# Bucketed attention with two MLPs: the clamp of the scores on VectorE becomes a row maximum, and ScalarE's exponential reads the scores from PSUM

## The chip, the cores and the metric

The kernel runs on one core of one Trainium2 chip. The metric is the device time of one execution in microseconds (us); the median of three runs stands for it. A core has TensorE (matrix products and transposes into PSUM, called PE), VectorE (DVE), ScalarE (ACT), GpSimd (POOL), and SyncE (SP), which here only starts DMA transfers. Each engine runs its own instructions in order, and the engines meet through semaphores.

## The reference, cut to what matters

```
mask   = q_bucket[:, :, :, None] == k_bucket[:, :, None, :]      # buckets: signs of 6 projections
scores = scale * q @ k.T ;  scores = where(mask, scores, -1e9)
scores = scores - max(scores, axis=-1) ;  attn = exp(scores) / (sum(exp(scores)) + 1e-9)
x = (attn @ v)  as (B*S, H*D)            # B 2, H 8, S 768, D 64
x = rational(x @ w_in0) @ w_out0         # 1536 x 512 -> 2048 -> 512, a cubic over a quadratic
x = (h * relu6(h + 3) / 6) @ w_out1      # h = x @ w_in1, the same sizes
```

A query whose bucket holds no key has -1e9 in its whole row, so its attention is uniform.

## The kernel before, in words

There are 16 heads, taken as 8 pairs, and each head has 6 tiles of 128 queries by 768 keys: 96 tiles, numbered n here, with j = 0 to 11 inside a pair and t = 0 to 5 inside a head. The 96 tiles are 96 steps, written out by hand in the same order on every engine. What one tile goes through is:

- **scores (L799 to L813)**: PE computes a tile of scores into one of two PSUM buffers (`s_ps`, by j % 2) with four products. Queries and keys are split in a high and a low part. The bits of the bucket stand as extra rows of `q_main` and `k_main`, so that a query and a key in different buckets get 2^33 per differing bit. All signs are turned: `q_main` and `q_cross` hold queries times -1/8 (`scale_col`), so the wanted maximum is a minimum.
- **clamp (L603)**: DVE reads the tile, takes the smaller of it and 1e9, writes it to `probs` in SBUF, and gets the row minimum (`least`) as accumulator output. `scores(n)` waits for `clamped` of tile n-2, since it writes the same buffer.
- **exponentials (L430)**: ACT computes exp(least - probs) in place in `probs`, with the row sum.
- **invert (L611)** on DVE, **normalise (L386)** on POOL: probs times 1 / row sum. `alone` is a wait followed by an increment of a semaphore that nobody reads.
- **turn_probs (L815)**: PE transposes tile n-3 in two halves of three 128 x 128 blocks; `take_turned` on ACT (first half) and on DVE (second half) copies them to SBUF.
- **weigh (L823)**: PE multiplies the transposed tiles of the pair before with v, spread over the steps: two k-blocks at t = 3, one at t = 1, 2, 4 and 5, none at t = 0. The first pair has no weigh at all. `upper_x` (ACT) and `lower_x` (DVE) split the result into `x_hi` and `x_lo`, which frees the bank for the next group.

A step on PE is: scores(n), a part of weigh, at j = 0 the projections of the next pair (`project`), then turn_probs(n-3). A step on DVE is: clamp(n), invert(n-1), at t = 0 lower_x, take_turned(n-3), at j = 1 `threshold` (the bits of the next pair), at t = 3 `split_lo` (the low parts of head h+2). A step on ACT is: at t = 0 upper_x, exponentials(n-1), take_turned(n-3), at t = 2 `split_hi` of head h+2, and in pairs 3 to 6 at j = 7 and j = 10 the high part of a weight (`split_weights`). A step on POOL is: normalise(n-1), and in pairs 3 to 6 at j = 8 and j = 11 the low part of a weight. In the last pair weigh is placed by `LAST_WEIGH` (L50): none at j = 0, 5, 10 and 11.

After the 96 steps the two MLPs follow in three chunks of 512 tokens each, with PE products back to back (L842 to L911). The diff does not touch them. Their first hidden products wait for the last exponentials and share PSUM banks with the scores.

Of the kernel before, what the change touches and what calls it, by code (L numbers as in the profile page):

```python
# [23 lines left out]
ALU = mybir.AluOpType  # L24
# [5 lines left out]
PENALTY = 2.0 ** 33  # L30
MASKED = 1e9


def bucket_attention_and_two_mlps(nc, q, k, v, proj, w_in0, w_out0, poly_a, poly_b, w_in1, w_out1, out):
# [57 lines left out]
    with ctx:  # L92
# [19 lines left out]
        three_col = sb("three_col", [P, 1])  # L112
        least = sb("least", [P, 4])
        scale_col = sb("scale_col", [P, 1])
        row_sum = sb("row_sum", [P, 4])
# [50 lines left out]
        sel_made = sem("sel_made")  # L166
        scale_made = sem("scale_made")
        proj_made = sem("proj_made")
# [13 lines left out]
        scored = sem("scored")  # L182
        clamped = sem("clamped")
        exped = sem("exped")
# [172 lines left out]
        def _(pool):  # L357
# [7 lines left out]
            def below(c, limit, fill):  # L365
# [5 lines left out]
            nc.gpsimd.memset(bit_sel[:, 0, :], TINY).then_inc(sel_made, 1)  # L371
            nc.gpsimd.memset(bit_sel[:, 1, :], -1.0).then_inc(sel_made, 1)
            pool.wait_ge(sel_made, 2)
# [3 lines left out]
            below(0, 3 * BITS, TINY)  # L377
            below(1, QUAD, -1.0)
            nc.gpsimd.memset(ident[:, :], 0.0).then_inc(sel_made, 1)
# [3 lines left out]
            nc.gpsimd.affine_select(out=ident[:, :], in_=ident[:, :], compare_op=ALU.not_equal, fill=1.0,  # L383
                                    base=0, pattern=[[-1, P]], channel_multiplier=1).then_inc(sel_made, 1)

            def normalise(n, j):  # L386
# [12 lines left out]
            for i in range(PAIRS):  # L399
                for j in range(2 * TILES):  # L400
                    n = 2 * TILES * i + j
                    if n >= 1:
                        normalise(n - 1, j - 1)
                    if early_half(i, j - 1):
                        f, half = early_half(i, j - 1)
                        split_weights(0, f, (half,))
# [8 lines left out]
        def _(act):  # L415
# [6 lines left out]
            def split_hi(h):  # L422

                i, u = divmod(h, 2)
                act.wait_ge(raw_in[i % 2][u], 32 * (i // 2 + 1))
                after(act, scored, TILES * (h - SETS + 1))
                nc.scalar.activation(q_main[h % SETS][:, :], raw[i % 2][u][:, :], ACT.Identity,
                                     scale=scale_col[:, 0:1]).then_inc(hi_made, 1)

            def exponentials(n, j):  # L430
                r = j % 4
                act.wait_ge(clamped, n + 1)
                nc.scalar.activation(probs[r][:, :], probs[r][:, :], ACT.Exp, scale=-1.0, bias=least[:, r:r + 1],  # L433
                                     accum_out=row_sum[:, r:r + 1]).then_inc(exped, 1)
# [141 lines left out]
        def _(dve):  # L576
            nc.vector.memset(proj_pair[:, :], 0.0).then_inc(proj_made, 1)
            nc.vector.memset(scale_col[0:D, :], -SCALE).then_inc(scale_made, 1)
            nc.vector.memset(scale_col[D:P, :], 1.0).then_inc(scale_made, 1)
            dve.wait_ge(proj_in, 32)  # L580
# [14 lines left out]
            def split_lo(h):  # L595

                c = h % SETS
                dve.wait_ge(hi_made, h + 1)
                nc.vector.scalar_tensor_tensor(q_cross[c][:, :], raw[h // 2 % 2][h % 2][:, :], scale_col[:, 0:1],
                                               q_main[c][:, :].bitcast(F32), ALU.mult, ALU.subtract)\  # L600
                    .then_inc(lo_made, 1)

            def clamp(n, j):  # L603

                r = j % 4
                dve.wait_ge(scored, n + 1)
                after(dve, turned, 2 * (n - 3))
                nc.vector.tensor_scalar(probs[r][:, :], s_ps[j % 2][:, 0:SEQ], MASKED, None, ALU.min, ALU.min,  # L608
                                        accum_out=least[:, r:r + 1]).then_inc(clamped, 1)

# [21 lines left out]
            def step(i, j):  # L632
                h, n = 2 * i + j // TILES, 2 * TILES * i + j
                t = j % TILES
                clamp(n, j)
                if n >= 1:
# [9 lines left out]
                if t == 3 and h + 2 < NHEAD:  # L646
# [3 lines left out]
            nc.vector.tensor_reduce(bit_col[:, :], bit_sel[:, :, :], AX.X, ALU.min).then_inc(bit_col_made, 1)  # L650
            dve.wait_ge(scale_made, 2)
            dve.wait_ge(raw_in[0][0], 32)
            nc.vector.tensor_scalar(q_main[0][:, :], raw[0][0][:, :], scale_col[:, 0:1], None, ALU.mult)\
                .then_inc(first_q, 1)
            dve.wait_ge(first_q, 1)
# [4 lines left out]
            dve.wait_ge(swapped_in, 32)  # L660
            nc.vector.tensor_scalar(q_cross[0][D:P, :], swapped[D:P, :], -SCALE, None, ALU.mult).then_inc(first_q, 1)
            nc.vector.scalar_tensor_tensor(q_cross[0][0:D, :], raw[0][0][0:D, :], -SCALE,
                                           q_main[0][0:D, :].bitcast(F32), ALU.mult, ALU.subtract).then_inc(first_q, 1)
            dve.wait_ge(first_q, 4)
# [117 lines left out]
        def _(pe):  # L782
# [16 lines left out]
            def scores(h, i, u, n, j, t):  # L799
# [5 lines left out]
                if n == 0:  # L805
                    pe.wait_ge(first_k, 2)
                after(pe, clamped, n - 1)
                rows = slice(P * t, P * (t + 1))
# [157 lines left out]
```

## Time and profile before

| | us |
|---|---|
| median of 3 runs | 774.07 (773.98 to 776.07) |
| the profiled execution, its own time | 773.98 |
| its span | 772.2 |
| PE busy | 751.7 (97%) |
| DVE busy | 484.8 (63%) |
| ACT busy | 431.7 (56%) |
| POOL busy | 170.0 (22%) |

The profile was taken from one execution. Its span leaves 1.8 us of that execution's time outside. A busy share is an average over stages: attention takes the first 240 us, the first MLP the stretch to about 510 us, the second one the rest. In the chain of work that ended last PE has 93% of the span.

### The profile page before, as it was taken

What the parts mean: (1) busy time and instruction counts of PE and PEld (TensorE: products, weight loads), DVE (VectorE), ACT (ScalarE), POOL (GpSimd) and SP (SyncE); (2) the same over time, 40 slices, a digit from 0 to 9 for tenths busy, and PEclk for the clock granted to TensorE, in tenths of its full rate; (3) what the DMA queues carried; (4) which work ended last, traced back from release to release, by engine and by line L of the source; (5) the groups of instructions that cost most, each with busy time, mean ns of one, the idle gap of its engine ahead of it and who ended that gap; (6) DMA issues with size and microseconds to landing.
All of it is one profiled execution on the core that took longest, in us unless ns stands there. A gap on an engine that the chain in (4) does not pass through costs nothing.

```text
span 772.2 us, 10988 instructions
## 1 busy us (share of the span) xinstructions
PE 751.7 (97%) x3712; PEld 580.0 (75%) x3712; DVE 484.8 (63%) x892; ACT 431.7 (56%) x783; POOL 170.0 (22%) x174
## 2 busy tenths in 40 slices
PE   4799999999999999999999999999999999999998
PEld 2666666666666888888888888888888888888886
DVE  4977777777766788899888998852222322232223
ACT  2866676776756888777676889852222221212121
POOL 0433344544531354200000244530000000000000
PEclk9999999999999999999999999999999999999999
DMA  6644355445300333100000133320000100010001
GB/s 149 161 119 108 89 135 136 94 108 126 80 27 1 83 86 105 56 0 0 0 0 0 42 96 109 89 76 0 1 1 0 54 0 0 0 55 0 1 1 55
DMA packets 35082, 43.29 MB, mean 56 GB/s; under 512 B 4192, under 2 KB 23392, under 8 KB 35040
## 3 DMA queue, kind: packets, MB, share of 16 engines
q1 hardware_dynamic: 34752, 42.32, 20.5%
q10 hardware_dynamic: 288, 0.43, 0.2%
q8 instruction: 24, 0.39, 0.2%
q14 instruction: 18, 0.15, 0.1%
HBM read 26.61 MB, written 3.15 MB: 39 GB/s over the span
## 4 chain that ended last, share of the span: by engine, by line
PE 93%; DVE 3%; DMA 1%; ACT 1%; issue 1%; SPq 1%; ACTq 0%; DVEq 0%
PE y_ps L911 34%; PE h_ps L857 11%; PE h_ps L858 11%; PE h_ps L859 11%; PE o_ps L837 9%; PE t_ps L820 8%; PE s_ps L810 3%; PE s_ps L811 3%; DVE probs L608 2%; DMA probs<-in_k 1%; DVE x_lo L629 1%; PE p_ps L794 1%; PE p_ps L837 1%; ACT probs L433 1%; DMA k_cross<-q_cross 0%
## 5 line engine op out<-in xcount | busy, mean ns | idle before, releaser
L703 DVE SCALAR_TENSOR_TENSOR t_abs<-t_abs,h_ps 128x512 f32<-128x512 f32 x48 | 33.0, 688 | 187.2 <-ACT t_abs L504 187.2
L857 PE MATMUL h_ps<-x_hi,slot 128*128 (+1 forms) x384 | 149.7, 390 | 0.0
L858 PE MATMUL h_ps<-x_lo,slot 128*128 (+1 forms) x384 | 149.4, 389 | 0.0
L859 PE MATMUL h_ps<-x_hi,slot 128*128 (+1 forms) x384 | 149.4, 389 | 0.0
L504 ACT ACTIVATE t_abs<-h_ps,three_col 128x512 f32<-128x512 f32 x48 | 33.1, 690 | 191.8 <-PE h_ps L859 191.8
L396 POOL TENSOR_TENSOR slot<-w_raw,slot 128x512 fp32r<-128x512 f32 x64 | 81.6, 1295 | 207.7 <-ACT slot L459 207.7
L911 PE MATMUL y_ps<-g_hi,slot 128*128 128x512 f32 x384 | 126.1, 389 | 0.0
L911 PE MATMUL y_ps<-slot,g_hi 128*128 128x512 f32 x384 | 118.3, 389 | 0.0
L389 POOL TENSOR_SCALAR probs<-probs,row_inv 128x768 f32<-128x768 f32 x96 | 87.2, 908 | 138.4 <-DVE row_inv L613 138.0
L820 PEld LDWEIGHTS t_ps<-ident,probs 128*128 128x128 f32 x576 | 61.9, 141 | 51.6 <-issue 34.3
L608 DVE TENSOR_SCALAR_CACHE_REDUCE probs<-s_ps 128x768 f32<-128x768 f32 x96 | 91.6, 954 | 12.6 <-PE s_ps L811 6.2
L433 ACT ACTIVATE probs<-probs,least 128x768 f32<-128x768 f32 x96 | 89.4, 931 | 10.8 <-DVE probs L608 10.7
L820 PE MATMUL t_ps<-ident,probs 128*128 128x128 f32 x576 | 84.1, 281 | 4.4 <-DVE pt_second L623 2.0
L857 PEld LDWEIGHTS h_ps<-x_hi,slot 128*128 128x128 f32 x384 | 72.1, 188 | 15.6 <-issue 0.6
L911 PEld LDWEIGHTS y_ps<-g_hi,slot 128*128 128x128 f32 x384 | 72.1, 188 | 15.3 <-DVE g_lo L709 0.2
L911 PEld LDWEIGHTS y_ps<-slot,g_hi 128*128 128x128 f32 x384 | 72.1, 188 | 14.9
L859 PEld LDWEIGHTS h_ps<-x_hi,slot 128*128 128x128 f32 x384 | 72.1, 188 | 14.9
L858 PEld LDWEIGHTS h_ps<-x_lo,slot 128*128 128x128 f32 x384 | 72.1, 188 | 14.8
L810 PE MATMUL s_ps<-k_cross,q_cross 128*128 128x512 f32 x192 | 74.3, 387 | 3.7 <-DMA k_main<-bits 2.9
L911 PE MATMUL y_ps<-g_lo,slot 128*128 128x512 f32 x192 | 74.7, 389 | 0.0
L911 PE MATMUL y_ps<-slot,g_lo 128*128 128x512 f32 x192 | 74.7, 389 | 0.0
L837 PE MATMUL o_ps<-pt_first,v_nat 128*64 128x384 f32 x180 | 72.8, 506 | 1.8 <-DVE x_lo L629 1.8
(72 smaller groups left out, 1097.9 us busy)
## 6 DMA issues: line engine op xcount, KB each, us to landing
w_raw<-in_moe_w_in SPq DMA_DIRECT2D x32, 256.0 KB, 2.7
w_raw<-in_moe_w_out SPq DMA_DIRECT2D x32, 256.0 KB, 2.7
raw<-in_q SPq DMA_DIRECT2D x16, 192.0 KB, 3.2
v_nat<-in_v SPq DMA_DIRECT2D x16, 192.0 KB, 3.1
raw<-in_k SPq DMA_DIRECT2D x15, 192.0 KB, 3.5
k_main<-q_main SPq DMA_DIRECT2D x15, 192.0 KB, 2.6
k_cross<-q_main SPq DMA_DIRECT2D x15, 192.0 KB, 3.1
k_cross<-q_cross SPq DMA_DIRECT2D x15, 192.0 KB, 2.6
```

Source lines behind the costliest of these rows:

```text
L389: nc.gpsimd.tensor_scalar(probs[j % 4][:, :], probs[j % 4][:, :], row_inv[:, r:r + 1], 1.0, ALU.mult, ALU.mult).then_inc(normed, 1)
L396: nc.gpsimd.tensor_tensor(slots[f][:, j, 1, :], w_raw[j][:, :], slots[f][:, j, 0, :].bitcast(F32), ALU.subtract).then_inc(w_lo_made, 1)
L433: nc.scalar.activation(probs[r][:, :], probs[r][:, :], ACT.Exp, scale=-1.0, bias=least[:, r:r + 1], accum_out=row_sum[:, r:r + 1]).then_in ...
L504: nc.scalar.activation(t_abs[b][:, :], h_ps[b][:, :], ACT.Relu, bias=three_col[:, :])\
L608: nc.vector.tensor_scalar(probs[r][:, :], s_ps[j % 2][:, 0:SEQ], MASKED, None, ALU.min, ALU.min, accum_out=least[:, r:r + 1]).then_inc(cla ...
L810: mm(s_ps[j % 2][:, c0:c1], q_cross[c][:, rows], k_cross[c][:, c0:c1], start=True, stop=False)
L820: last = nc.tensor.transpose(t_ps[half][:, P * s:P * (s + 1)], probs[n % 4][:, c:c + P], ident[:, :])
L837: last = mm(weigh_bank(e)[D * u:D * (u + 1), 0:HALF], v_nat[i % 2][u][:, kt, :], pt(i, u, g)[:, kt, :], start=(kt == 0), stop=(kt == TILES ...
L857: mm(h_ps[b][:, :], w_hi, x_hi[:, kt, cols], start=(kt == 0), stop=False)
L858: mm(h_ps[b][:, :], w_hi, x_lo[:, kt, cols], start=False, stop=False)
L859: last = mm(h_ps[b][:, :], w_lo, x_hi[:, kt, cols], start=False, stop=(kt == KT - 1))
L911: last = mm(y_ps[d][:, :], still, moving, start=(f == 0 and a == 0), stop=(f == FT - 1 and a == 2))
```

## The change: what it does

The signs are turned back: queries are copied unscaled, the bits of the query side are 1 instead of -1, and the score is large and negative outside the bucket. DVE no longer rewrites the tile: `maximum(n)` reads the PSUM buffer and writes one number per row, minus the row maximum (`neg_max`). Two new POOL instructions of one column, `bias(n)`, stand ahead of normalise(n-1) in POOL's order: the first makes `exp_scale` = 1/8 where the row has a key in its bucket (`neg_max` under 2^32) and 0 where not, the second makes `exp_bias` = `neg_max` times `exp_scale`. ACT's exponential now reads the scores in PSUM, with both as operands of one number per row, and writes `probs`. It takes over the wait for a free `probs` buffer (tile n-4 transposed). `scores(n)` waits for `exped` of tile n-2 instead of `clamped`. `split_hi` becomes a copy without a scale, `split_lo` a subtraction without one; two memsets of `scale_col` go. MATCHED is 2^32.

```diff
-MASKED = 1e9
+MATCHED = PENALTY / 2
@@ POOL
-            nc.gpsimd.memset(bit_sel[:, 1, :], -1.0).then_inc(sel_made, 1)
+            nc.gpsimd.memset(bit_sel[:, 1, :], 1.0).then_inc(sel_made, 1)
-            below(1, QUAD, -1.0)
+            below(1, QUAD, 1.0)
+            def bias(n, j):
+                r = j % 4
+                neg = neg_max[:, r:r + 1]
+                alone(maxed, n + 1)
+                nc.gpsimd.tensor_scalar(exp_scale[:, r:r + 1], neg, MATCHED, SCALE, ALU.is_lt, ALU.mult)\
+                    .then_inc(matched, 1)
+                alone(matched, n + 1)
+                nc.gpsimd.tensor_scalar(exp_bias[:, r:r + 1], neg, exp_scale[:, r:r + 1], 1.0, ALU.mult, ALU.mult)\
+                    .then_inc(biased, 1)
...
+                    bias(n, j)
                     if n >= 1:
                         normalise(n - 1, j - 1)
@@ ACT
-                nc.scalar.activation(q_main[h % SETS][:, :], raw[i % 2][u][:, :], ACT.Identity,
-                                     scale=scale_col[:, 0:1]).then_inc(hi_made, 1)
+                nc.scalar.activation(q_main[h % SETS][:, :], raw[i % 2][u][:, :], ACT.Copy).then_inc(hi_made, 1)
...
-                act.wait_ge(clamped, n + 1)
-                nc.scalar.activation(probs[r][:, :], probs[r][:, :], ACT.Exp, scale=-1.0, bias=least[:, r:r + 1],
+                act.wait_ge(biased, n + 1)
+                after(act, turned, 2 * (n - 3))
+                nc.scalar.activation(probs[j % 4][:, :], s_ps[j % 2][:, 0:SEQ], ACT.Exp,
+                                     scale=exp_scale[:, r:r + 1], bias=exp_bias[:, r:r + 1],
                                      accum_out=row_sum[:, r:r + 1]).then_inc(exped, 1)
@@ DVE
-                nc.vector.scalar_tensor_tensor(q_cross[c][:, :], raw[h // 2 % 2][h % 2][:, :], scale_col[:, 0:1],
-                                               q_main[c][:, :].bitcast(F32), ALU.mult, ALU.subtract)\
-                    .then_inc(lo_made, 1)
+                nc.vector.tensor_tensor(q_cross[c][:, :], raw[h // 2 % 2][h % 2][:, :], q_main[c][:, :].bitcast(F32),
+                                        ALU.subtract).then_inc(lo_made, 1)
...
-            def clamp(n, j):
-                r = j % 4
-                dve.wait_ge(scored, n + 1)
-                after(dve, turned, 2 * (n - 3))
-                nc.vector.tensor_scalar(probs[r][:, :], s_ps[j % 2][:, 0:SEQ], MASKED, None, ALU.min, ALU.min,
-                                        accum_out=least[:, r:r + 1]).then_inc(clamped, 1)
+            def maximum(n, j):
+                dve.wait_ge(scored, n + 1)
+                nc.vector.tensor_reduce(neg_max[:, j % 4:j % 4 + 1], s_ps[j % 2][:, 0:SEQ], AX.X, ALU.max,
+                                        negate=True)\
+                    .then_inc(maxed, 1)
@@ PE
-                after(pe, clamped, n - 1)
+                after(pe, exped, n - 1)
```

The four instructions with which DVE makes the first head's operands lose their scale in the same way (a copy or a plain subtraction in place of each).

## Rows read from the trace of the kernel before

**Rows 1.** Busy time by stretch: busy us of each engine, clock, DMA share, GB/s.
```profile
20.00:30.00 10.00, 7.18 (x47) 6.00 (x48) 9.56 (x22) 7.50 (x16) 4.67 (x6) 1.00 0.67 181
70.00:100.00 30.00, 29.77 (x189) 19.28 (x187) 23.18 (x56) 20.64 (x43) 11.81 (x13) 1.00 0.45 112
```
**Rows 2.** Timeline of PE, first pair: start, us, then the instruction.
```profile
21.88 0.50 PE L810 MATMUL s_ps<-k_cross,q_cross 128*128 128x512 f32 x1 [0.83 <-DVE probs L608]
...
28.23 0.48 PE L810 MATMUL s_ps<-k_cross,q_cross 128*128 128x512 f32 x1
...
29.74 0.48 PE L810 MATMUL s_ps<-k_cross,q_cross 128*128 128x512 f32 x1
...
37.32 0.48 PE L810 MATMUL s_ps<-k_cross,q_cross 128*128 128x512 f32 x1
```
**Rows 3.** Timeline of DVE, first pair.
```profile
20.87 0.95 DVE L608 TENSOR_SCALAR_CACHE_REDUCE probs<-s_ps 128x768 f32<-128x768 f32 x1
...
22.92 0.16 DVE L613 RECIPROCAL row_inv<-row_sum 128x1 f32<-128x1 f32 x1 [0.16 <-ACT probs L433]
...
23.45 1.55 DVE L599 SCALAR_TENSOR_TENSOR q_cross<-raw,scale_col,q_main 128x768 fp32r<-128x768 f32 x1
24.93 0.94 DVE L608 TENSOR_SCALAR_CACHE_REDUCE probs<-s_ps 128x768 f32<-128x768 f32 x1
...
30.73 0.96 DVE L608 TENSOR_SCALAR_CACHE_REDUCE probs<-s_ps 128x768 f32<-128x768 f32 x1
```
**Rows 4.** Timeline of ACT, DVE and POOL around one exponential.
```profile
45.40 0.92 ACT L433 ACTIVATE probs<-probs,least 128x768 f32<-128x768 f32 x1
46.45 0.17 DVE L613 RECIPROCAL row_inv<-row_sum 128x1 f32<-128x1 f32 x1 [0.27 <-ACT probs L433]
46.81 0.91 POOL L389 TENSOR_SCALAR probs<-probs,row_inv 128x768 f32<-128x768 f32 x1 [1.40 <-DVE row_inv L613]
```
**Rows 5.** Timeline of POOL at the start: small instructions.
```profile
0.82 0.10 POOL L372 MEMSET bit_sel<- 128x4 f32 x1
0.99 0.19 POOL L367 TENSOR_SCALAR_AFFINE_SELECT bit_sel<-bit_sel 128x4 f32<-128x4 f32 x1
...
2.15 0.29 POOL L383 TENSOR_SCALAR_AFFINE_SELECT ident<-ident 128x128 f32<-128x128 f32 x1
```
**Rows 6.** Groups by line and shape, 36 to 268 us: count, busy us, mean ns.
```profile
L389 POOL TENSOR_SCALAR probs<-probs,row_inv 128x768 f32<-128x768 f32 x87 | 79.0, 908 | 114.4 <-DVE row_inv L613 113.9
...
L501 ACT ACTIVATE t_num<-h_ps,a_col 128x512 f32<-128x512 f32 x5 | 3.8, 765 | 0.0
...
L500 ACT ACTIVATE r_ps<-h_ps 128x512 f32<-128x512 f32 x5 | 3.0, 591 | 0.0
```
**Rows 7.** Timeline of DVE at the start: a single-source operation on 768 columns.
```profile
5.63 0.62 DVE L653 TENSOR_SCALAR q_main<-raw,scale_col 128x768 fp32r<-128x768 f32 x1 [1.75 <-DMA raw<-in_k]
```
**Rows 8.** Timeline of DVE, PE and ACT, second head of pair 1.
```profile
48.86 0.95 DVE L608 TENSOR_SCALAR_CACHE_REDUCE probs<-s_ps 128x768 f32<-128x768 f32 x1
...
51.78 0.48 PE L810 MATMUL s_ps<-k_cross,q_cross 128*128 128x512 f32 x1
...
52.49 0.94 ACT L433 ACTIVATE probs<-probs,least 128x768 f32<-128x768 f32 x1
...
53.16 0.47 PE L810 MATMUL s_ps<-k_cross,q_cross 128*128 128x512 f32 x1
...
54.34 0.54 PE L837 MATMUL o_ps<-pt_first,v_nat 128*64 128x384 f32 x1 [0.23 <-DVE x_lo L629]
55.77 0.48 PE L810 MATMUL s_ps<-k_cross,q_cross 128*128 128x512 f32 x1
56.66 0.54 PE L837 MATMUL o_ps<-pt_first,v_nat 128*64 128x384 f32 x1
```
**Rows 9.** Waits of PE in all: us in total, times, longest.
```profile
PE o_ps L837 <- DVE x_lo L629: 1.8, 8, 0.2
```
**Rows 10.** Timeline of PE at the end of attention.
```profile
233.11 0.47 PE L810 MATMUL s_ps<-k_cross,q_cross 128*128 128x512 f32 x1
```

More of the change, by code:

```diff
@@ L112, in bucket_attention_and_two_mlps @@
         three_col = sb("three_col", [P, 1])
-        least = sb("least", [P, 4])
-        scale_col = sb("scale_col", [P, 1])
+        neg_max = sb("neg_max", [P, 4])
+        exp_scale = sb("exp_scale", [P, 4])
+        exp_bias = sb("exp_bias", [P, 4])
         row_sum = sb("row_sum", [P, 4])
@@ L166, in bucket_attention_and_two_mlps @@
         sel_made = sem("sel_made")
-        scale_made = sem("scale_made")
         proj_made = sem("proj_made")
@@ L182, in bucket_attention_and_two_mlps @@
         scored = sem("scored")
-        clamped = sem("clamped")
+        maxed = sem("maxed")
+        matched = sem("matched")
+        biased = sem("biased")
         exped = sem("exped")
@@ L577, in _ @@
             nc.vector.memset(proj_pair[:, :], 0.0).then_inc(proj_made, 1)
-            nc.vector.memset(scale_col[0:D, :], -SCALE).then_inc(scale_made, 1)
-            nc.vector.memset(scale_col[D:P, :], 1.0).then_inc(scale_made, 1)
             dve.wait_ge(proj_in, 32)
@@ L634, in step @@
                 t = j % TILES
-                clamp(n, j)
+                maximum(n, j)
                 if n >= 1:
@@ L650, in _ @@
             nc.vector.tensor_reduce(bit_col[:, :], bit_sel[:, :, :], AX.X, ALU.min).then_inc(bit_col_made, 1)
-            dve.wait_ge(scale_made, 2)
             dve.wait_ge(raw_in[0][0], 32)
-            nc.vector.tensor_scalar(q_main[0][:, :], raw[0][0][:, :], scale_col[:, 0:1], None, ALU.mult)\
-                .then_inc(first_q, 1)
+            nc.vector.tensor_copy(q_main[0][:, :], raw[0][0][:, :]).then_inc(first_q, 1)
             dve.wait_ge(first_q, 1)
@@ L660, in _ @@
             dve.wait_ge(swapped_in, 32)
-            nc.vector.tensor_scalar(q_cross[0][D:P, :], swapped[D:P, :], -SCALE, None, ALU.mult).then_inc(first_q, 1)
-            nc.vector.scalar_tensor_tensor(q_cross[0][0:D, :], raw[0][0][0:D, :], -SCALE,
-                                           q_main[0][0:D, :].bitcast(F32), ALU.mult, ALU.subtract).then_inc(first_q, 1)
+            nc.vector.tensor_copy(q_cross[0][D:P, :], swapped[D:P, :]).then_inc(first_q, 1)
+            nc.vector.tensor_tensor(q_cross[0][0:D, :], raw[0][0][0:D, :], q_main[0][0:D, :].bitcast(F32),
+                                    ALU.subtract).then_inc(first_q, 1)
             dve.wait_ge(first_q, 4)
```

## The prediction

> **What bounds the kernel now.** I read the busy shares by stretch first. From 70 to 100 us, which stands for pairs 1 to 7, PE is busy 29.77 us of 30; in the first pair, 20 to 30 us, it is 7.18 of 10 while DVE has 9.56 [rows 1]. So attention has two regimes: a first pair without weigh, bound by DVE and by the passing of tiles between engines, and seven pairs bound by PE. Behind attention PE runs without gaps, with products the diff doesn't touch; what attention loses is not made up there. Then I read timelines, to see what each tile waits for. Scores of one tile start at 28.23 us and of the next at 29.74: 1.5 us a step where nothing special intervenes [rows 2]. In the steady part a usual step is 2.3 us long, but the second head's first tile, at 51.78, has no weigh and is followed by the next at 53.16, after 1.38 us [rows 8].
>
> **The new loop.** A PSUM buffer used to be free when DVE had clamped it. Now scores(n+2) waits for scores(n), row maximum, two POOL instructions and exponential in series. Its terms:
>
> - Start of scores to start of DVE's pass: 29.74 to 30.73, 0.99 us [rows 2, 3].
> - The pass: the clamp takes 0.95 [rows 3]. No reduction of that size from PSUM is in the trace. It reads the same 768 columns, so I take 0.95 again; the lower bound is the 0.62 of a single-source pass over 768 columns in SBUF [rows 7], the upper about 1.0.
> - POOL, from the end of the pass to the start of the exponential, called E. DVE to POOL through `alone`: the reciprocal ends at 46.62, normalise starts at 46.81, 0.19 [rows 4]. POOL has no one-column tensor_scalar to read. Below it stands a memset of 0.10; a select of 4 columns takes 0.19 and one of 128 columns 0.29 [rows 5]. That slope, 0.10 over 124 columns, makes 0.62 over 768, so of the 0.908 of normalise [rows 6] at most 0.29 is fixed cost. I take 0.22 an instruction, near the 4-column select. Between the two, POOL waits for itself: 0.07 from the memset's end at 0.92 to the select at 0.99 [rows 5] at least, 0.19 at most; I take 0.12. To ACT 0.05. Sum: 0.19 + 0.22 + 0.12 + 0.22 + 0.05 = 0.80. The ends are 0.19 + 0.10 + 0.07 + 0.10 + 0.05 = 0.51 and 0.19 + 0.29 + 0.19 + 0.29 + 0.08 = 1.04.
> - The exponential until PE may start: 45.40 to 46.45 when the reciprocal starts behind it, 1.05 [rows 4]. The second one-number-per-row operand adds: a pass over 512 columns takes 0.591 without any and 0.765 with two [rows 6], 0.087 each. So 1.05 + 0.08 = 1.13.
>
> Loop: 0.99 + 0.95 + 0.80 + 1.13 = 3.87 us for two steps, 1.93 from the end of the maximum. Where two steps on PE take less, PE waits.
>
> The Trainium skill, GPSIMD Engine Reference, section 3.1 on cycle accounting, has one- and two-operation bodies at 1.03 cycles per element at 1.2 GHz. By that, 768 columns are 0.66 us of the 0.908 and 0.25 is fixed, an estimate from that page; E would be 0.86 and the loop 3.93. No run here shows which of the two splits holds.
>
> **First pair.** Before, tile 2's clamp starts at 20.87, held up by the threshold that waits for a DMA, and scores of tile 4 start at 21.88 [rows 2, 3]. Nothing before that moves the 20.87. After: 20.87 + 0.95 = 21.82, plus 1.93 gives 23.75, 1.9 us late. Next, DVE's split_lo at t = 3 stands behind invert(2), which needs exponential 2: 21.82 + 0.80 + 1.05 = 23.67, where it was 22.92. From that reciprocal to the next clamp are 2.01 us (22.92 to 24.93), in which split_lo takes 1.55 [rows 3]. So maximum 4 starts at 25.68, ends at 26.63, and tile 6 starts at 28.56. Two loops later tile 10 starts at 28.56 + 7.74 = 36.30. For tile 12: tile 8 starts at 32.43, its exponential at 32.43 + 0.99 + 0.95 + 0.80 = 35.17, the reciprocal at 36.22, maximum 10 at 38.23 (split_lo again), its end 39.18, and tile 12 at 41.11. It was 37.32 [rows 2]: **+3.8 us**. E enters five times: the low end gives 2.3, the high end 5.0. The odd tiles stand between: their bias is queued behind a normalise of 0.91 on POOL, which delays it past the even tile's, but a loop of theirs is as long, so they follow at the same period. Up to 1.0 goes off if split_lo doesn't meet POOL's normalise as it seems to now (twice some 0.5).
>
> **Pairs 1 to 7.** A usual pair of steps on PE is 4.6 us, over the 3.87: no wait. Two places are tight. First, the short step: the exponential at 52.49 is held by ACT's own queue (copy, upper_x), not by E (tile j = 5's maximum would be ready at 51.41 + 0.80). Scores at 53.16 must now wait for it: 52.49 + 1.13 = 53.62, 0.46 late. The weigh behind starts 0.89 after its scores (55.77 to 56.66), so at 54.51; it stood at 54.34 because it waited 0.23 for x_lo [rows 8]. That leaves 0.17. PE has 8 such waits [rows 9], one a pair and a second in the last: 8 x 0.17 = **+1.4**. The ninth short step ends at 233.11 [rows 10] with no weigh behind it: its 0.46 falls partly into waits for DVE's copies at the end; I take **+0.2**. Second, the tile after split_lo: its maximum starts at 48.86 and ends at 49.81; + 1.93 is 51.74, and its PE step starts at 51.78 [rows 8]. That costs nothing, with 0.04 of room, twice in each pair. With E at 1.04 it costs 0.2 each of 14 times, 2.8.
>
> **The rest.** normalise(n-1) stands behind bias(n), but its reciprocal stood behind clamp(n) on DVE anyway; it comes 0.6 us later and is wanted two steps later, over 3 us in the short case: nothing. The POOL weight splits in pairs 3 to 6 delay the next bias by some 0.5, in steps with 0.7 of room: nothing. ACT's split_hi loses an operand (0.087) and DVE's split_lo too; they are off the path except once ahead of the first scores: -0.1. DVE loses the write of probs, which nobody waits for. SP's queue keeps its order; its key and bit transfers start up to 2 us later in the first pair, with several in hand. The last exponential is 0.9 later, and the last transposes stand behind 3 us of hidden products and a whole weigh. DVE's four first-head instructions: 0 within 0.1.
>
> Sum: 3.8 + 1.4 + 0.2 - 0.1 = +5.3 us on an execution of 773.98 (the median is 774.07, the same within 0.1): **779.3 us**. Own range, by E, the pass and the split_lo meeting: 776.6 to 783.
>
> **Rivals.**
>
> *POOL's small instructions are dearer, E about 1.04.* First pair +5.0, the tight places after split_lo +2.8, short steps as before 1.5: 783.3. For: normalise allows 0.29 fixed. Against: the 4-column select at 0.19. It decides above E = 0.84. Chance 0.17.
>
> *Not slower: the chain shrinks under DVE's own pace.* If the reduction, which writes no tile, runs like the 0.62 row less its fixed part, say 0.55, with E at 0.51 and the exponential at 1.05 (its PSUM source paying for the operand), the loop is 0.99 + 0.55 + 0.51 + 1.05 = 3.10, 1.55 a step against 1.5. invert(2) is then at 22.90, no later than now, tile 12 about 0.2 late; the short steps give 8 x 0.08 = 0.6. Place: the maximum and POOL; point: a loop under some 3.2 us. Time 774.7. Against: 0.95 for the clamp of the same tile. Chance 0.10. The Trainium skill, VectorE: DVE Perf Modes, the perf-mode tier table, gives tensor_reduce only the single rate, SBUF or PSUM; by it the pass stays at 0.95 and this case loses its main term. No row here shows a long reduction.
>
> *PE slows in the thinner first pair.* The granted clock reads 1.00 there [rows 1], but PE would be busy some 6 of 10 us. If products fall to half speed, scores take 0.65 more in each of five loops: +3.3, 782.6. Against: at 7.18 of 10 they stay at 0.48. Chance 0.06.
>
> **How the numbers follow.** Forecast 0.64, the three rivals 0.17, 0.10 and 0.06, unnamed gains 0.03. A measurement of this kernel tells about 0.3%, 2.3 us, from no change. Slower by more: forecast 0.62, rivals 0.23, so 0.85. Within: 0.02 of the forecast's low end and the not-slower rival, 0.12. Faster 0.03. Range 776.3 to 783.6.
>
> **What would show it.** Right: PE waiting for ACT at the scores of the first pair; two even tiles 3.9 us apart there; tile 12 at about 41 us; PE waiting for ACT 0.46 once a pair, at the second head's second tile, and a weigh behind it without a wait for DVE; POOL's two instructions near 0.2 each and 0.8 from L608's successor to the exponential; the MLPs' length unchanged. Wrong: waits of PE in usual steps or after split_lo (E too low), a reduction far from 0.95, or a first pair that ends before 39 us. The forecast falls if the first pair's period stays near 1.5.

## The result, and the profile after

The changed kernel takes **782.49 us** (782.09 to 783.22 over four runs), the kernel before 774.05 beside it (773.98 to 776.07). The ratio is 1.0103, 95% interval 1.009 to 1.0115: slower by 8.4 us. The prediction was 779.3, range 776.3 to 783.6. The sign and most of the places were right, and the size was too small by 3.2 us. The profiled execution spans 780.8 us, 8.6 more than that of before.

The table follows one thing through attention: by how much scores of a tile start later than in the kernel before. Each entry is the difference of two start times in the two timelines of PE. "Key split" is short for `split_lo`, the DVE instruction `q_cross<-raw,q_main`, which makes the low parts of a later head; it stands twice in each pair, in the last pair not at all. A "short step" is a step of PE without a weigh: one in each of pairs 1 to 6, at the pair's middle, and two in the last pair before its end.

| Where | later by, us | forecast |
|---|---|---|
| tile 12 (end of the first pair) | 4.40 | 3.8 |
| six short steps, pairs 1 to 6, after the weigh: 0.20 to 0.23 each | +1.36 | 6 x 0.17 = 1.0 |
| tile behind the second key split of a pair, pairs 1 and 2: 0.10 each | +0.20 | 0 |
| the same place, pairs 3 to 6: 0.44, 0.40, 0.43, 0.45 | +1.73 | 0 |
| last pair, its two short steps | +0.6 | 0.3 |
| end of attention | +0.4 | 0.2 |

The entries add up to 8.7 and the span grew by 8.6: between these places single tiles drift back by some hundredths. The tile behind the first key split of each pair is 0.10 late as well, but the short step comes right behind it and swallows that: its exponential is held by ACT's own queue, so the step costs 0.20 to 0.23 with that delay (here) and without it (experiment 1). Everything after attention has the length it had, 535.8 us from the first hidden product to the end against 535.7.

The two stretches of the busy table, to be held against [rows 1]; the columns are window, length, busy us of PE, PEld, DVE, ACT and POOL, granted clock, DMA share, GB/s:

```profile
20.00:30.00 10.00, 8.48 (x38) 7.33 (x39) 7.40 (x14) 6.54 (x13) 6.47 (x13) 1.00 0.66 181
70.00:100.00 30.00, 29.87 (x190) 19.32 (x191) 22.87 (x43) 21.66 (x45) 17.44 (x40) 1.00 0.41 98
```

DVE, which was 9.56 busy of the first ten, is now 7.40 busy. The first pair is no longer bound by one engine but by the series of PE, DVE, POOL and ACT that each buffer passes through. PE does fewer instructions in the same ten microseconds (38 against 47) and is busier: some of them ran at half rate, on which more below.

The loop of the first pair, in the timelines of POOL and ACT, and PE's answer to it [rows 2]:

```profile
26.85 0.23 POOL L394 TENSOR_SCALAR exp_scale<-neg_max 128x1 f32<-128x1 f32 x1 [0.68 <-DVE neg_max L618]
27.28 0.27 POOL L397 TENSOR_SCALAR exp_bias<-neg_max,exp_scale 128x1 f32<-128x1 f32 x1 [0.20 <-POOL exp_scale L394]
...
27.58 0.99 ACT L448 ACTIVATE probs<-s_ps,exp_bias,exp_scale 128x768 f32<-128x768 f32 x1 [0.75 <-POOL exp_bias L397]
...
28.81 0.47 PE L819 MATMUL s_ps<-k_cross,q_cross 128*128 128x512 f32 x1 [0.43 <-ACT probs L448]
```

From the exponential's start to PE's is 28.81 - 27.58 = 1.23 here; in most tiles of the first pair it is 1.13. The reduction before it starts at 25.70 and ends at 26.65, so E, from the end of the maximum to the exponential, is 27.58 - 26.65 = 0.93. It reads 0.92 to 0.93 wherever nothing else holds the exponential. The groups by shape give the parts:

```profile
L448 ACT ACTIVATE probs<-s_ps,exp_bias,exp_scale 128x768 f32<-128x768 f32 x96 | 95.0, 990 | 32.9 <-POOL exp_bias L397 31.5
L618 DVE TENSOR_REDUCE neg_max<-s_ps 128x1 f32<-128x768 f32 x96 | 91.6, 954 | 18.1 <-PE s_ps L820 15.0
...
L397 POOL TENSOR_SCALAR exp_bias<-neg_max,exp_scale 128x1 f32<-128x1 f32 x96 | 26.2, 273 | 19.9 <-POOL exp_scale L394 17.1 <-DVE row_inv L624 2.8
L394 POOL TENSOR_SCALAR exp_scale<-neg_max 128x1 f32<-128x1 f32 x96 | 21.6, 225 | 81.2 <-DVE neg_max L618 79.9
```

The short step, beside [rows 8]: scores at 56.34 and then 58.09, where 51.78 and 53.16 stood, and a weigh with no bracket behind it, so nothing to wait for.

```profile
56.34 0.47 PE L819 MATMUL s_ps<-k_cross,q_cross 128*128 128x512 f32 x1
...
56.95 1.00 ACT L448 ACTIVATE probs<-s_ps,exp_bias,exp_scale 128x768 f32<-128x768 f32 x1
...
58.09 0.51 PE L819 MATMUL s_ps<-k_cross,q_cross 128*128 128x512 f32 x1
...
59.01 0.54 PE L846 MATMUL o_ps<-pt_first,v_nat 128*64 128x384 f32 x1
```

PE's waits in all: the row of [rows 9], for x_lo, is gone, and this one has come.

```profile
PE s_ps L819 <- ACT probs L448: 6.1, 13, 1.3
```

**What the prediction called nothing.** Beside the ninth tile of a pair POOL splits a half of the next weights (L410), in pairs 3 to 6 only. POOL first, then DVE:

```profile
121.43 1.27 POOL L410 TENSOR_TENSOR slot<-w_raw,slot 128x512 fp32r<-128x512 f32 x1
122.67 0.23 POOL L394 TENSOR_SCALAR exp_scale<-neg_max 128x1 f32<-128x1 f32 x1
123.10 0.26 POOL L397 TENSOR_SCALAR exp_bias<-neg_max,exp_scale 128x1 f32<-128x1 f32 x1 [0.20 <-POOL exp_scale L394]
123.33 0.91 POOL L403 TENSOR_SCALAR probs<-probs,row_inv 128x768 f32<-128x768 f32 x1
```
```profile
123.77 1.28 DVE L613 TENSOR_TENSOR q_cross<-raw,q_main 128x768 fp32r<-128x768 f32 x1
124.97 0.94 DVE L618 TENSOR_REDUCE neg_max<-s_ps 128x1 f32<-128x768 f32 x1
```

The weight split pushes the one-column instructions, and behind them normalise, back by 0.47 (held against the same place of pair 2, where normalise starts 0.92 ahead of the key split and here 0.44). DVE's key split begins at 123.77 while normalise runs until 124.24, and takes 1.28 instead of 0.95. This is called the meeting below. The next reduction starts 0.34 later for it, and the tile that waits for that reduction has no room.

### The profile page after: what moved, and what is told of

Same layout as the page of the kernel before. It is cut to its first block, busy times and chain, and to the rows that moved or that the text cites. A ratio compares the mean times of both kernels' runs of the same rounds, so it can differ in the third digit from the quotient of the medians.

```text
span 780.8 us, 11273 instructions
## 1 busy us (share of the span) xinstructions
PE 759.1 (97%) x3712; PEld 583.4 (75%) x3712; DVE 486.0 (62%) x794; ACT 439.5 (56%) x783; POOL 215.3 (28%) x366
## 4 chain that ended last, share of the span: by engine, by line
PE 89%; issue 2%; DVE 2%; ACT 2%; DMA 1%; POOL 1%; SPq 1%; ACTq 0%; POOLq 0%; DVEq 0%
PE y_ps L920 33%; PE h_ps L866 11%; PE h_ps L867 11%; PE h_ps L868 11%; PE o_ps L846 8%; PE t_ps L829 7%; PE s_ps L819 4%; PE s_ps L820 3%; ACT probs L448 2%; DVE neg_max L618 1%; DMA probs<-in_k 1%; PE p_ps L803 1%; DVE q_cross L613 1%; PE p_ps L846 1%; POOL exp_bias L397 0%
## 5 line engine op out<-in xcount | busy, mean ns | idle before, releaser
L410 POOL TENSOR_TENSOR slot<-w_raw,slot 128x512 fp32r<-128x512 f32 x64 | 81.6, 1293 | 207.0 <-ACT slot L475 206.9
L448 ACT ACTIVATE probs<-s_ps,exp_bias,exp_scale 128x768 f32<-128x768 f32 x96 | 95.0, 990 | 32.9 <-POOL exp_bias L397 31.5
L618 DVE TENSOR_REDUCE neg_max<-s_ps 128x1 f32<-128x768 f32 x96 | 91.6, 954 | 18.1 <-PE s_ps L820 15.0
L829 PEld LDWEIGHTS t_ps<-ident,probs 128*128 128x128 f32 x576 | 63.5, 143 | 46.4 <-issue 26.2
L846 PE MATMUL o_ps<-pt_second,v_nat 128*64 128x384 f32 x180 | 72.9, 506 | 0.0
```

What stands on the lines that cost most here:

```text
L410: nc.gpsimd.tensor_tensor(slots[f][:, j, 1, :], w_raw[j][:, :], slots[f][:, j, 0, :].bitcast(F32), ALU.subtract).then_inc(w_lo_made, 1)
L448: nc.scalar.activation(probs[j % 4][:, :], s_ps[j % 2][:, 0:SEQ], ACT.Exp, scale=exp_scale[:, r:r + 1], bias=exp_bias[:, r:r + 1], accum_o ...
L618: nc.vector.tensor_reduce(neg_max[:, j % 4:j % 4 + 1], s_ps[j % 2][:, 0:SEQ], AX.X, ALU.max, negate=True)\
L829: last = nc.tensor.transpose(t_ps[half][:, P * s:P * (s + 1)], probs[n % 4][:, c:c + P], ident[:, :])
L846: last = mm(weigh_bank(e)[D * u:D * (u + 1), 0:HALF], v_nat[i % 2][u][:, kt, :], pt(i, u, g)[:, kt, :], start=(kt == 0), stop=(kt == TILES ...
```

## The experiments

Two theories at the start. **A:** the loop through the exponential is on the path in the first pair and at a few tight steps, its length is E plus fixed parts, and DVE and POOL hold each other up where they meet. **B:** the loss comes from what the change adds to the engines (POOL's work, the dearer exponential), wherever it stands. The kernel before stood at 774.0 to 774.1 beside all of them. What no experiment varied by itself is the exponential's new source and second operand, which together make it 0.06 longer.

**1. One POOL instruction instead of two.** The scale is a constant; the test of the masked rows is left out.

```diff
+            nc.gpsimd.memset(exp_scale[:, :], SCALE).then_inc(matched, 1)
-                nc.gpsimd.tensor_scalar(exp_scale[:, r:r + 1], neg, MATCHED, SCALE, ALU.is_lt, ALU.mult)\
-                    .then_inc(matched, 1)
-                alone(matched, n + 1)
```

> The changed kernel with one POOL instruction in bias instead of two: exp_scale is filled with 1/8 once, exp_bias is neg_max times it, so a row without any key in its bucket is no longer made uniform (left out); ACT still takes both operands from SBUF. Latency theory: E falls from the measured 0.93 us to 0.50, since one instruction (0.225 us) and one wait of POOL for itself (0.20) go. The first pair gains 5 x 0.43 = 2.1, the steps after split_lo 0.1 each (7 times), and the normalise in pairs 3 to 6 comes early enough not to meet split_lo (4 x 0.34 = 1.4): 782.5 - 4.2 = 778.3, between 777.5 and 779.5. Rival, that waiting for the exponential at all costs the time and POOL's part is small: 782 to 781.5, and then the kernel before with that wait alone is near 781. Rival, that the time goes with POOL's occupancy: a gain by its share, half of the 8.4, in all steps evenly, with no pattern in the short steps.

Measured: 779.26 (779.13 to 779.59), ratio 1.0059 [1.0046, 1.0073]. E reads 0.50, the hand-over from DVE and this one instruction:

```profile
49.72 0.27 POOL L397 TENSOR_SCALAR exp_bias<-neg_max,exp_scale 128x1 f32<-128x1 f32 x1 [0.83 <-DVE neg_max L618]
```

Tile 12 is 3.34 late instead of 4.40, and at the pairs' ends the key split reads 0.95 and costs nothing. That is what A says, a microsecond dearer than expected. The trace shows where most of it went: in the first pair both key splits now start 0.17 behind a normalise and take 1.54, where they took 0.95 in the changed kernel. The shorter E moved normalise ahead of them. The second of the two:

```profile
36.35 0.91 POOL L403 TENSOR_SCALAR probs<-probs,row_inv 128x768 f32<-128x768 f32 x1
...
36.52 1.54 DVE L613 TENSOR_TENSOR q_cross<-raw,q_main 128x768 fp32r<-128x768 f32 x1
```

Tile 10's reduction starts 1.98 behind its scores for that and not 1.38, tile 4's 1.98 and not 1.69: 0.9 in all. In its first pair the granted clock falls too; of its five runs the four with a mean clock of 0.996 took 779.13 to 779.30 and the one at 1.000 took 779.59, so the fall, as far as that number shows it, isn't what the microsecond went to.

```profile
22.00:26.00 4.00, 3.22 (x13) 2.63 (x12) 3.31 (x5) 2.62 (x6) 2.28 (x4) 0.50 0.86 227
```

**2. The same two instructions on DVE.** Nothing left out.

```diff
@@ POOL
-                    bias(n, j)
@@ DVE
+                dve.wait_ge(maxed, n + 1)
+                nc.vector.tensor_scalar(exp_scale[:, r:r + 1], neg, MATCHED, SCALE, ALU.is_lt, ALU.mult)\
+                    .then_inc(matched, 1)
+                dve.wait_ge(matched, n + 1)
+                nc.vector.tensor_scalar(exp_bias[:, r:r + 1], neg, exp_scale[:, r:r + 1], None, ALU.mult)\
+                    .then_inc(biased, 1)
```

> The changed kernel with both small instructions on DVE, right behind the maximum, and POOL left with normalise. Latency theory: E is 0.06 + 0.16 + 0.06 + 0.16 + 0.05, about 0.5 as with one POOL instruction, so the first pair gains 2.1 and the steps after split_lo and the meetings of split_lo with POOL another 2.1; against it DVE's lower_x stands 0.3 later in the short steps, where weigh waits for it, up to 8 x 0.15 = 1.2. About 779, between 778 and 780. Rival, that reading PSUM from ACT or the wait for the exponential is what costs: stays at 782. Rival, that DVE has no room in the first pair: no gain there, and tile 12 starts at 41.7 as now.

Measured: 783.39 (783.28 to 783.55), ratio 1.0112 [1.0097, 1.0128]: a miss by 4. E is 0.47 as expected (0.154 and 0.214 for the instructions), but the path has moved. DVE's x_lo now stands behind both instructions, and the weigh at the short step waits for it again:

```profile
58.74 0.50 PE L814 MATMUL s_ps<-k_cross,q_cross 128*128 128x512 f32 x1 [0.23 <-ACT probs L435]
...
59.28 0.54 DVE L635 TENSOR_TENSOR x_lo<-o_ps,x_hi 128x384 fp32r<-128x384 f32 x1
...
59.88 0.54 PE L841 MATMUL o_ps<-pt_first,v_nat 128*64 128x384 f32 x1 [0.16 <-DVE x_lo L635]
```

Each short step costs 0.42 to 0.45 here instead of 0.20 to 0.23. In the first pair both key splits meet a normalise and take 1.54, as in experiment 1. And PE, after idling before tile 12, does tile 12 at half rate (tile 13 is 5.08 late where tile 12 is 3.56):

```profile
41.00:44.00 3.00, 3.00 (x13) 1.35 (x14) 2.30 (x9) 1.20 (x3) 0.90 (x1) 0.50 0.35 77
```

So the path through E got shorter by 0.46 and the kernel no faster: what DVE took over it owed to x_lo and to the key splits.

**3. The kernel before with the new wait alone.** Clamp, operands and engines as before; PE waits for the exponential.

```diff
-                after(pe, clamped, n - 1)
+                after(pe, exped, n - 1)
```

> The kernel before with one edit: scores(n) waits for exped of tile n-2 instead of clamped, which nothing in it needs. Latency theory: the loop is 0.99 + 0.95 + 0.05 + 1.05 = 3.04 us for two steps, just over DVE's own 2.9. Tile 4 starts 1.0 later, of which DVE's queue swallows most by tile 6; tile 12 is 0.5 late; the short steps cost 0.38, 0.1 behind the wait for x_lo, 8 times. About 775.3, between 774.6 and 776.3. Rival, that the longer hold of the PSUM buffer is the whole cost whatever stands in the loop: 780 or more.

Measured: 776.50 (775.83 to 776.67), ratio 1.0024 [1.0015, 1.0033]. That is 0.2 above the expected range. With no POOL instruction added and the short exponential, the wait by itself costs 2.4 us: 1.25 in the first pair, where 0.5 was expected, and 0.14 to 0.16 at each short step of pairs 1 to 6. B, by which nothing has been added here, can't explain these. For the other 6 us of the change it is the places that speak against B: the losses of the table stand at single tiles, and the tiles between them, which have the same added work, lose nothing. Those 6 us hang on E, on the exponential's 0.06, and on what they push together. The granted clock falls to 0.50 in this profile's first pair, and what that has in the 1.25 stays open.

**4. Without the weight split that stands beside the pair's end.** Zeros are written in place of the low parts of the first halves of the early weights, so those residuals are missing from the products.

```diff
+                    if m == 0 and f < EARLY_SLOTS and j == 0:
+                        nc.gpsimd.memset(slots[f][:, 0, 1, :].bitcast(F32), 0.0).then_inc(w_lo_made, 1)
+                        continue
```

> The changed kernel with POOL's first early weight split of pairs 3 to 6 (0.5 us of memset to zero in place of the 1.28 us subtraction, so the low parts of the first four input weights are left out). Theory of the meeting: the 1.28 us delay bias and normalise by 0.45, normalise then runs into DVE's split_lo, which takes 1.28 instead of 0.95, and tile 0 of the next pair starts 0.43 late instead of 0.09. So 4 x 0.34 = 1.4 goes: 781.1, and split_lo reads 0.95 at about 123.8. Rival, that the 0.43 comes from POOL's second split or from ACT's weight copies in these pairs: unchanged at 782.5.

Measured: 781.71 (780.64 to 783.07), ratio 1.0087 [1.0073, 1.01]. The median is 0.8 below the changed kernel's and the runs are wide apart, so the time alone decides little; the trace does. It is of the slowest of the five runs (783.07, clock 0.991): tile 13 is 6.08 late where it was 4.42, with PE at half rate for some 10 us of the first pair and again at its end. From tile 13 to the start of the last pair it then loses 1.89 where the changed kernel loses 3.19, so 1.3 is saved, near the 1.4 expected. The key split in pair 3, where 1.28 stood:

```profile
125.42 0.95 DVE L616 TENSOR_TENSOR q_cross<-raw,q_main 128x768 fp32r<-128x768 f32 x1
```

It is 0.95 at all four places, and the tiles behind are later by 0.10 to 0.12 instead of 0.40 to 0.45.

**5. The same weight split, one step later.** Nothing left out.

```diff
-    EARLY_AT = (7, 10)
+    EARLY_AT = (8, 10)
```

> The changed kernel with POOL's first early split of the next weights issued beside tile j=9 instead of j=8 (the second stays where it is). Changed kernel 782.5. Theory (in pairs 3 to 6 the weight split of 1.27 us on POOL delays the one-column operation and the normalise of tile 9, and DVE's key split then runs into the normalise: 1.28 instead of 0.95, so the next pair begins 0.43 late instead of 0.09): if DVE's key split gets in ahead of the weight split, each of four pairs gives back 0.34, 1.4 in all: 781.1. If the weight split gets in ahead, the key split waits for all of it and reads up to 2.2, about 1.2 more at each of four pairs: 787. Rival (the 0.43 at these places has another cause, such as the transfers of the next weights): 782.5 either way, the key split still 1.28.

Measured: 781.95 (781.45 to 782.57), ratio 1.01 [1.0084, 1.0115], between the expectations. DVE and POOL at the same place:

```profile
124.38 1.05 DVE L613 TENSOR_TENSOR q_cross<-raw,q_main 128x768 fp32r<-128x768 f32 x1
```
```profile
124.60 1.98 POOL L410 TENSOR_TENSOR slot<-w_raw,slot 128x512 fp32r<-128x512 f32 x1
126.56 0.22 POOL L394 TENSOR_SCALAR exp_scale<-neg_max 128x1 f32<-128x1 f32 x1
```

The key split got in first and its 1.28 became 1.05. But the weight split that now starts behind it takes 1.98 instead of 1.27, and the bias of tile 46, whose reduction ended at 126.30, has to wait for its end; that costs 0.06. The four places cost 0.26, 0.30, 0.25 and 0.30: 0.6 less than in the changed kernel in all, of the 1.4 hoped for. What is left of the meeting is the key split's 0.10 to 0.13 and the 0.06 of the bias; the larger part of the delay now falls on the weight split, which nobody waits for.

**6. PE kept busy in the first pair of the changed kernel.** Extra transposes into a PSUM tile that nobody uses there.

```diff
+                if i == 0:
+                    for _ in range(12 if n == 2 else 4):
+                        nc.tensor.transpose(o_ps[:, 0:P], ident[:, :], ident[:, :])
```

> The changed kernel with extra transposes of the identity on TensorE into a PSUM tile that the first pair does not use: four per step of the first pair and 12 at its second step; nothing left out. Theory of the clock (PE stood idle before tiles 3 and 4, whose products then ran at half rate, 1.69 instead of 0.99 from the scores to the reduction): with PE kept busy the two tiles run at full rate, first pair about 0.3 to 1.0 us shorter, 781.5 to 782.2, and the runs of one kernel lie closer together. Rival (the late tiles come from the chain DVE, POOL, ACT alone): 782.5 or a little above, since the extra transposes can only delay products. If the transposes delay products by 0.1 at each of ten steps: 783.5.

Measured: 782.54 (781.96 to 782.68), ratio 1.0107 [1.0092, 1.0123]: no gain. In both kernels PE begins attention at half rate. Before, the products of tile 3 are at full rate; in the changed kernel, where PE idled 1.34 us before tile 3, those of tiles 3 and 4 are not. A product by the main keys in tile 3 of the kernel before; then tile 3's start and tile 4 of the changed kernel; then tile 4 of this one:

```profile
19.31 0.40 PE L811 MATMUL s_ps<-k_main,q_main 76*128 76x512 f32 x1
```
```profile
20.99 0.80 PE L819 MATMUL s_ps<-k_cross,q_cross 128*128 128x512 f32 x1 [1.34 <-ACT probs L448]
...
24.01 0.80 PE L819 MATMUL s_ps<-k_cross,q_cross 128*128 128x512 f32 x1
24.61 0.63 PE L820 MATMUL s_ps<-k_main,q_main 76*128 76x512 f32 x1
```
```profile
23.96 0.51 PE L819 MATMUL s_ps<-k_cross,q_cross 128*128 128x512 f32 x1 [0.84 <-ACT probs L448]
24.31 0.40 PE L820 MATMUL s_ps<-k_main,q_main 76*128 76x512 f32 x1
```

So the half rate was real and the transposes took it away: tile 5 starts at 25.80 instead of 26.60. The 0.80 is given back at once. DVE's key split now falls beside a normalise that started at 24.31, ahead of it, takes 1.54 and not 0.95, and tile 6 starts at 29.04 against 28.81; tile 12 starts at 41.86, against 41.72.

```profile
24.48 1.54 DVE L613 TENSOR_TENSOR q_cross<-raw,q_main 128x768 fp32r<-128x768 f32 x1
```

**7. The same transposes in the kernel before.**

> The kernel before with the same extra transposes in the first pair. Theory of the clock: 774.0 in every run, with none at 776, and a granted clock of 1.0; the median not lower than before by more than 0.3. Rival (the runs at 776 have another cause): one run in five or so still at 776. If the transposes themselves are in the way of products: 774.5 to 775.

Measured: 775.64 over eleven runs (775.37 to 775.99), ratio 1.0019 [1.001, 1.0028]. The clock is 0.999 or 1.0 in each run and none stands apart, as the theory had it; but it is 1.6 slower, which none of the expectations held. The reason is in PE's timeline:

```profile
28.82 0.60 PE L878 MATMUL o_ps<-ident 128*128 128x128 f32 x4
29.18 0.48 PE L810 MATMUL s_ps<-k_cross,q_cross 128*128 128x512 f32 x1
...
30.98 0.48 PE L810 MATMUL s_ps<-k_cross,q_cross 128*128 128x512 f32 x1
```

With four more transposes a step PE is full, and a step takes 1.80 us where DVE's pace was 1.5 [rows 2].

**8. A third POOL instruction in the chain.** The scale times 1.0; nothing left out.

```diff
-                alone(matched, n + 1)
+                alone(matched, 2 * n + 1)
+                nc.gpsimd.tensor_scalar(exp_scale[:, r:r + 1], exp_scale[:, r:r + 1], 1.0, 1.0, ALU.mult, ALU.mult)\
+                    .then_inc(matched, 1)
+                alone(matched, 2 * n + 2)
```

> The changed kernel with a third one-column operation on POOL in the chain from the maximum to the exponential (the exponent's scale times 1.0, nothing left out). By the changed kernel's trace such an operation takes 0.23 after a wait for POOL's own result of 0.20, so the chain goes from 0.93 to 1.36. Theory (the chain is on the path in the first pair and at the tight steps): first pair five exponentials on the path, +2.1; the tile behind each key split, already late by 0.09 at 0.93, late by all of the 0.43 more at some 13 places, +5.6; the short steps at the pair's middle +0.3 each, +1.8 of which some is the same slack: 790 to 792. Rival (only the six or seven short steps and the first pair see the chain): +2.1 and 7 times 0.43, 787.5. If the chain were hidden in the steady loop: 784.6.

Measured: 798.63 (797.82 to 799.33), ratio 1.0314 [1.03, 1.0328]: dearer than any expectation, 16.1 over the changed kernel. E is 1.31, 0.38 more (the instruction takes 0.19, its wait 0.20). A tile behind each key split is late by 0.7 to 1.0, not by 0.4. POOL, DVE and PE in pair 1:

```profile
71.30 0.91 POOL L406 TENSOR_SCALAR probs<-probs,row_inv 128x768 f32<-128x768 f32 x1
71.53 1.48 DVE L616 TENSOR_TENSOR q_cross<-raw,q_main 128x768 fp32r<-128x768 f32 x1
...
76.42 0.47 PE L822 MATMUL s_ps<-k_cross,q_cross 128*128 128x512 f32 x1 [0.78 <-ACT probs L451]
```

A longer E pushes normalise into the key split: at 8 of the 12 places behind the first pair it takes 1.19 to 1.48 instead of 0.95; at the other four it comes first, and POOL's last bias instruction takes 0.96 to 0.98 instead of 0.26. The meeting adds itself to the wait. But the key splits are only half of the 16.8 by which this span exceeds the changed kernel's. By PE's timeline the twelve places lose 8.5 more than there. The first pair up to tile 13 loses 4.1 more, 1.5 of it because PE does tile 12 at half rate (granted clock 0.50 from 45.5 to 47.5). And at the start of pairs 4, 5 and 6 the bias now has to wait for POOL's second weight split, which costs 0.7 each; so it does, for 0.9, in the last pair. What is left stands in the last pair and at the end of attention. In pair 4:

```profile
138.79 1.28 POOL L413 TENSOR_TENSOR slot<-w_raw,slot 128x512 fp32r<-128x512 f32 x1
140.06 0.22 POOL L394 TENSOR_SCALAR exp_scale<-neg_max 128x1 f32<-128x1 f32 x1
...
142.31 0.50 PE L822 MATMUL s_ps<-k_cross,q_cross 128*128 128x512 f32 x1 [0.41 <-ACT probs L451]
```

**9. Only eight extra transposes, in the kernel before**, behind the scores of tiles 2 and 3.

```diff
+                if i == 0:
+                    for _ in range(4 if n in (2, 3) else 0):
+                        nc.tensor.transpose(o_ps[:, 0:P], ident[:, :], ident[:, :])
```

> The kernel before with four extra transposes of the identity behind the scores of tiles 2 and 3 alone, where PE otherwise idles before tile 4 at 21.88 us. The warmed version of before gave 775.64 with no run apart from the others (775.37 to 775.99) and cost its 1.6 because four transposes lengthened every step of the first pair. Theory (the runs of before at 776 are those in which PE's products fall to half rate after the idle time around 20 us): with the transposes there alone, no run at 776 and a median of 774.0 to 774.5. If half-rate products cost something in the ordinary runs of before too: 773.5. Rival (the extra transposes cost by being there, or the runs at 776 come from elsewhere in the first pair): 775 or more, or one run in five still near 776.

Measured: 774.00 over eleven runs (773.83 to 774.15) beside 774.06 (773.76 to 776.0), ratio 0.9997 [0.9988, 1.0006]. The time is the theory's, its reason is not: the clock fell all the same, only later.

```profile
24.00:26.00 2.00, 2.00 (x9) 1.81 (x9) 2.00 (x4) 0.80 (x3) 0.33 (x1) 0.50 0.69 198
```

DVE is busy without a gap there, so slow products cost the kernel before little in that stretch: tile 5 is 0.70 late and tile 8 0.20. Of the 49 runs of the kernel before, five stood near 776 (776.00 to 776.12), 1.4 us or more from the rest; of the 22 with transposes, none stood apart from its own group. That is too few to call the cause shown. No version beat the kernel before.

**Time against E.** The experiments in one table, each against the kernel before beside it:

| kernel | E, us | slower by, us |
|---|---|---|
| before, waiting for the exponential | 0.05 | 2.4 |
| one POOL instruction | 0.50 | 5.2 |
| both instructions on DVE | 0.47 | 9.3 |
| changed kernel | 0.93 | 8.4 |
| three POOL instructions | 1.31 | 24.6 |

E alone doesn't give the time: of two kernels with E near 0.5 one is 4.1 slower than the other. Along the versions that keep the work on POOL or add none, a microsecond of E costs 6 to 7.5 up to 0.93, and the last 0.38 cost 16.2. The prediction put a step at E = 0.84, where the tile behind the key split runs out of room. The trace has it there: 0.10 at E = 0.93, nothing at 0.50. The 16.2 are more than that step, since a meeting at the key splits, a stretch at half rate and the weight splits come with it, and only one version stands beyond 0.93.

## Why the prediction was right in sign and short in size

- **The loop, right.** The maximum takes 0.954 for 0.95; from the exponential to PE it is 1.13 for 1.13; the exponential takes 0.990, 0.059 more than before, for 0.08. Tile 4 at 24.01 for 23.75, tile 6 at 28.81 for 28.56.
- **E, a term of the sum mis-sized: 0.93 for 0.80.** The second instruction takes 0.273 and not 0.22, POOL waits 0.20 for itself and not 0.12, the hand-over from DVE is about 0.2 as read [rows 4]. The four-column select [rows 5] was a good neighbour for the first instruction (0.225) and not for the second. The forecast's upper choice of 0.19 for the self-wait, which was in the range, was the right one. The Trainium skill, GPSIMD Engine Reference, section 3.1 (Elementwise: side-by-side cycle accounting), led to an estimate of 0.25 an instruction and E = 0.86; the trace's 0.225 and 0.273 average just that. The second of the rivals (not slower, by a pass of 0.55) had nothing in it: the pass is 0.954.
- **The first pair, 4.40 for 3.8.** Five times 0.13 is 0.65 and would give 4.45. That it came out so near is in part luck, since two further things cancelled: the key splits took 0.95 and not 1.55, and PE did tiles 3 and 4 at half rate, 0.70 longer each from scores to reduction (1.69 for 0.99). The third rival (chance 0.06) was thus half right, for two tiles and not five. Experiment 6 shows that taking the half rate away gains nothing: the key split then meets the normalise and takes its 1.54 again.
- **The short step, right:** PE is 0.47 late for 0.46 against the tiles before the pair's middle, and 0.20 to 0.23 is left after the weigh for 0.17.
- **The tile behind the key split.** The room was 0.04 and E came out 0.13 longer, so 0.09 were to be expected, and 0.10 came. A wait of PE behind `split_lo` was among the prediction's own signs of being wrong, and it appeared. The prediction counted 14 such places, but the last pair has no key split, so there are 12, and the first of each pair is swallowed by the short step; the dear-POOL rival's 2.8 for E = 1.04 was too high by that count.
- **The step that failed: "the POOL weight splits in pairs 3 to 6 delay the next bias by some 0.5, in steps with 0.7 of room: nothing."** The delay is 0.47 and the bias has room; normalise behind it does not matter for its own tile either. What was not asked is whom the late normalise runs into. It meets DVE's key split, whose delay goes to the next maximum, in a tile without room: 1.73 in four pairs where pairs 1 and 2 lose 0.10 each, so 1.3 us more. Experiment 4, without the weight split, and experiment 1, with a shorter E, both take it away; experiment 5 takes half of it.
- **The sum.** 0.6 more than forecast in the first pair, 0.3 in the short steps, 0.6 for the tiles behind the second key split by E alone (six times 0.10), 1.3 for the meetings, 0.5 in the last pair and the end: 3.3, for the 3.3 by which the span of 780.8 exceeds the forecast's 5.3 on 772.2. Of these the 1.3 come from the failed step, and the rest from E and from short-step costs that were put too low.

## What to carry to other kernels

When a buffer's release moves behind a chain of small instructions, price the chain by its hand-overs as well as by its instructions (0.20 each here), and list each step whose slack is smaller than what you don't know of the chain: those are the places where a longer chain first shows. When work on GpSimd moves by half a microsecond, look at which VectorE instruction with two SBUF inputs it now overlaps, since that decided more here than the delay itself. Taking one delay out (the half rate of PE, a POOL instruction, the weight split) can hand the time to the next meeting, so read the trace of the mended kernel before adding up gains.

## What the runs showed of the hardware

- **DVE and POOL hold each other up.** A key split with two inputs from SBUF takes 0.95; begun 0.44 behind a normalise it takes 1.28, 0.23 behind (experiment 8) 1.48, 0.17 behind (normalise at 24.31, experiment 6) 1.54. Where POOL's instruction is the later one, it is POOL's that is long: the weight split's 1.98 for 1.27 in experiment 5, the last bias instruction's 0.98 for 0.26 in experiment 8. In the changed kernel's first pair the two starts lie 0.04 apart, 24.49 for normalise and 24.53 for the key split, and there normalise is held, 1.68 for 0.91, while the key split takes its 0.95; which of the two got in first the trace doesn't show:

```profile
24.49 1.68 POOL L403 TENSOR_SCALAR probs<-probs,row_inv 128x768 f32<-128x768 f32 x1
```

  A held key split behaves as if it could begin only when normalise was done: it ends 0.81 after normalise's end (125.05 and 124.24), 0.80 (73.01 and 72.21) and, in experiment 5 with a normalise from 123.73 to 124.64, 0.79. The Trainium skill, GPSIMD Engine Reference, section 8 (Key points), says that GpSimd shares its SBUF interfaces with VectorE and contends with VectorE instructions that have two SBUF inputs. By that rule a key split and a normalise collide wherever they overlap; the trace agrees, with the amounts above.
- **The granted clock.** In the profiles of experiments 1 to 5, 8 and 9 it falls to 0.50, the 1.2 GHz level, for some 3 to 10 us in or just behind the first pair, each time after PE had idled; in experiments 2, 4 and 8 it does so twice. A product of 512 columns by the main keys then takes 0.63 instead of 0.40. In the changed kernel's own profile the column reads 1.00 while these products of tiles 3 and 4 take 0.63: the durations show the level there, the column does not.
- **One-column instructions.** On POOL 0.19 for a multiplication by two numbers written in the instruction (experiment 8), 0.225 for a compare and a multiplication by such numbers, 0.273 with one number per row as operand; on DVE the last two take 0.154 and 0.214 (experiment 2). Between two that depend on each other POOL waits 0.20.
